# Head 0's operands built from the masks' own raw tile, mask rows turned straight into place, and a last stage with its middle tap on ScalarE, its low parts on VectorE and three gate buffers

## The reference

```python
# 1: attention within clusters, for each of 2 x 8 heads of 768 x 64
q_assign = argmax(q_n @ c_n.T); k_assign = argmax(k_n @ c_n.T)     # 16 centroids, rows normalised
mask = q_assign[:, None] == k_assign[None, :]
scores = where(mask, q @ k.T / 8, -1e9)
x = softmax(scores) @ v
# 2: Fourier mixing over tokens and channels, then a two-layer MLP on the normalised sum
u = x + real(fft(fft(x, axis=1), axis=2)); un = layernorm(u)
x = u + relu(un @ w_ch1) @ w_ch2
# 3: gated layer with a convolution of 3 taps along the tokens
h = relu(x @ w_in)                                                # 2 x 768 x 1024
conv_out = conv_w[0] * h_left + conv_w[1] * h + conv_w[2] * h_right
out = (h * sigmoid(conv_out)) @ w_out
```

## Time and profile before

| | us |
|---|---|
| runs | 730.78, 731.47, 728.44 (median 730.78) |
| profiled execution, its own time | 728.22 |
| its span, first to last instruction | 726.4 |
| TensorE busy | 704.0 (97% of the span) |
| VectorE, ScalarE, GpSimd busy | 378.1, 289.9, 286.4 |
| granted TensorE clock, mean | 0.991 of full speed |

### The profile page before, as it was taken

One profiled execution on the slowest core, in us unless ns is written; L12 is line 12 of the kernel. 1 busy time (PEld: TensorE's weight loads), 2 busy tenths in 40 slices (PEclk: granted clock), 3 DMA queues, 4 the chain that ended last, 5 costly groups with the idle time before them and its releaser, 6 DMA issues.

```text
span 726.4 us, 10339 instructions
## 1 busy us (share of the span) xinstructions
PE 704.0 (97%) x3927; PEld 631.5 (87%) x3927; DVE 378.1 (52%) x704; ACT 289.9 (40%) x602; POOL 286.4 (39%) x305
## 2 busy tenths in 40 slices
PE   8899999999999999999999999999999999799998
PEld 8799999999999999988888888888888899688886
DVE  3688778788888883973312311132111378874410
ACT  2567667676767773211002110021001264443320
POOL 3466697588548606067820000000041247531100
PEclk8899999999999999999999999999999999999999
DMA  5525445242435202133300000000040331000011
GB/s 164 142 79 131 127 102 144 62 104 62 128 121 153 63 1 66 30 76 103 112 30 1 0 1 1 0 29 30 0 162 12 110 95 30 0 30 16 28 49 54
DMA packets 26865, 48.09 MB, mean 66 GB/s; under 512 B 4032, under 2 KB 11456, under 8 KB 26560
## 3 DMA queue, kind: packets, MB, share of 16 engines
q1 hardware_dynamic: 24240, 39.44, 19.7%
q0 software_dynamic: 2448, 7.95, 3.4%
q10 hardware_dynamic: 128, 0.05, 0.0%
HBM read 36.41 MB, written 3.15 MB: 54 GB/s over the span
## 4 chain that ended last, share of the span: by engine, by line
PE 77%; DVE 10%; ACT 8%; issue 2%; POOL 1%; DMA 1%; SPq 0%; ACTq 0%; POOLq 0%
PE ps L1508 18%; PE ps L1474 18%; PE ps L1570 9%; PE ps L1273 8%; PE ps L1259 6%; PE ps L1556 5%; ACT prob L674 3%; PE ps L1247 3%; PE ps L1248 3%; PE ps L1214 3%; ACT pt_h L686 2%; DVE pt_l L870 2%; DVE gate L1165 2%; DVE row_min L863 2%; PE ps L1353 1%
## 5 line engine op out<-in xcount | busy, mean ns | idle before, releaser
L1103 DVE SCALAR_TENSOR_TENSOR hid_l<-ps,hid_h 128x512 fp32r<-128x512 f32 x48 | 33.2, 692 | 197.2 <-ACT hid_h L772 197.2
L870 DVE TENSOR_TENSOR pt_l<-ps,pt_h 128x384 fp32r<-128x384 f32 x192 | 101.0, 551 | 47.1 <-ACT pt_h L686 46.0
L772 ACT ACTIVATE hid_h<-ps 128x512 fp32r<-128x512 f32 x48 | 28.7, 598 | 223.7 <-PE ps L1474 223.7
L686 ACT ACTIVATE pt_h<-ps 128x384 fp32r<-128x384 f32 x192 | 84.0, 490 | 56.6 <-PE ps L1259 56.5
L863 DVE TENSOR_REDUCE row_min<-ps 128x1 f32<-128x768 f32 x96 | 90.3, 940 | 8.1 <-PE ps L1248 8.1
L1259 PE MATMUL ps<-cst,prob 128*128 128x128 f32 x576 | 82.3, 280 | 9.5 <-ACT prob L674 9.5
L674 ACT ACTIVATE prob<-ps,row_min 128x768 f32<-128x768 f32 x96 | 87.3, 909 | 5.3 <-DVE row_min L863 4.9
L1259 PEld LDWEIGHTS ps<-cst,prob 128*128 128x128 f32 x576 | 65.4, 144 | 18.7 <-ACT prob L674 14.7
L1508 PE MATMUL ps<-w_h,hid_h 128*128 128x512 f32 x192 | 76.2, 397 | 0.0
L1508 PE MATMUL ps<-w_h,hid_l 128*128 128x512 f32 x192 | 75.5, 393 | 0.0
L1508 PE MATMUL ps<-w_l,hid_h 128*128 128x512 f32 x192 | 74.7, 389 | 0.0
(11 more groups left out here) (166 smaller groups left out, 1570.3 us busy)
## 6 DMA issues: line engine op xcount, KB each, us to landing
w_raw<-in_moe_w_ch SPq DMA_DIRECT2D x24, 256.0 KB, 2.6
raw_d<-in_q SPq DMA_DIRECT2D x8, 384.0 KB, 3.9
raw_d<-in_k SPq DMA_DIRECT2D x8, 384.0 KB, 5.6
raw_qk<-in_q SPq DMA_DIRECT2D x16, 192.0 KB, 4.9
raw_qk<-in_k SPq DMA_DIRECT2D x16, 192.0 KB, 3.2
raw_v<-in_v SPq DMA_DIRECT2D x16, 192.0 KB, 2.5
q<-q SPq DMA_DIRECT2D x16, 192.0 KB, 4.4
k<-k SPq DMA_DIRECT2D x16, 192.0 KB, 4.1
```

Of the source, the lines that this page charges most:

```text
L686: nc.scalar.activation(pt_h[a][:, R * hf:R * hf + R, (t % R) * P:(t % R + 1) * P], ps[:, 4 + hf, 0:HALF].rearrange("p (j c) -> p j c", j=R ...
L870: nc.vector.tensor_tensor(pt_l[a][part], ps[:, 4 + hf, 0:HALF].rearrange("p (j c) -> p j c", j=R), as_f32(pt_h[a][part]), ALU.subtract).th ...
```

## The change

**Head 0.** No DMA copy and no mask DMA serves head 0 any more. q and k of head 0 are rows 0 to 63 of the masks' raw tiles, so they aren't loaded a second time: GpSimd scales `raw_d[0]` into `raw_qk`, ScalarE writes the high part twice (into `q1` and `q2`) and the same for k, GpSimd takes both low parts. The raw k tile is now issued at the start of ScalarE's queue. The mask rows of head 0 are turned by `turn_rows`, 6 transposes for q and 6 for k, straight to partitions 0 to 15 of PSUM; ScalarE copies q's rows and half of k's into place, VectorE the other half. `keep_busy(12)` and `keep_busy(8)` have become `keep_busy(2)` and `keep_busy(4)`. An exponential that nobody reads brings ScalarE's table load forward. The dots and the masks of unit 1 move one step later against the steps of head 0.

**Last stage.** The middle tap is an activation with a scale on ScalarE (`middle_tap`), all low parts are VectorE's, GpSimd only splits `w_out`, now right at the start, from four raw buffers loaded earlier and one DMA for the high part; `act_s` and `gate` have three buffers, sigmoid, gate and low part follow one and two rounds behind.

```diff
-                        if n or j == 0:
-                            sp.dma_start(as_f32(mask_place(t, tp)), as_f32(rows_of(n, j, tp))).then_inc(done, 16)
+                        sp.dma_start(as_f32(mask_place(t, tp)), as_f32(rows_of(n, j, tp))).then_inc(done, 16)
...
+            sp.dma_start(raw_d[0][:, :], pair_of(q_t, 0)).then_inc(raw_d_loaded[0], 16)
+            load_k(0, 1)
             load_v(0, 0)
             sp.dma_start(taps[:, :, :], conv_w).then_inc(taps_loaded, 16)
+            sp.wait_ge(q2_first, 1)
+            sp.wait_ge(q_split, 1)
+            load_q(0, 1)
+            sp.wait_ge(k_high, 1)
+            sp.wait_ge(k_split, 1)
+            load_dots(1)
...
+            serve(0, 1)
+            for i in range(1, PAIRS - 1):
...
-            scale_q(0)
-            split_qk(0, 0)
+            pool.wait_ge(raw_d_loaded[0], 16)
+            nc.gpsimd.tensor_scalar(raw_qk[0:D, :], raw_d[0][0:D, :], -SCALE, 1.0, ALU.mult,
+                                    ALU.mult).then_inc(q_scaled, 1)
+            pool.wait_ge(q_scaled, 1)
+            pool.wait_ge(q_high, 1)
+            low(q1[0][D:P, :], raw_qk[0:D, :], as_f32(q1[0][0:D, :])).then_inc(q_split, 1)
+            pool.wait_ge(q_split, 1)
+            pool.wait_ge(k2_first, 1)
+            low(k1[0][0:D, :], raw_d[1][0:D, :], as_f32(k2[0][0:D, :])).then_inc(k_split, 1)
...
+            nc.gpsimd.dma_start(out_h[:, :, :], w_out.rearrange("(f p) c -> p f c", p=P)).then_inc(outw_high, 16)
+            pool.wait_ge(mlp_ready, B * NT)
...
+            for t in range(3):
+                step(0, 0, t)
             store_mask(1)
-            for t in range(2, 4):
-                step(0, 0, t)
+            step(0, 0, 3)
...
+            def middle_tap(n):
+                act.wait_ge(relu_done, 2 * n + 2)
+                if n >= 3:
+                    act.wait_ge(g_low, n - 2)
+                nc.scalar.activation(gate[n % 3][:, :], act_s[n % 3][:, 1:S + 1], ACT.Copy,
+                                     scale=taps[:, 1, n % FT2:n % FT2 + 1]).then_inc(tap_done, 1)
...
             for n in range(B * FT2):
                 rectify(n)
+                middle_tap(n)
                 if n >= 1:
-                    gate_high(n - 1)
+                    squash(n - 1)
+                if n >= 2:
+                    gate_high(n - 2)
...
             for n in range(B * FT2):
+                convolve(n)
                 if n >= 1:
                     apply_gate(n - 1)
-                convolve(n)
-                if n >= 1 and not low_by_pool(n - 1):
-                    gated_low(n - 1)
-                if 1 <= n < FT2:
+                if n >= 2:
+                    gated_low(n - 2)
+                if n < FT2:
...
+            def turn_rows(j):
+
+                pe.wait_ge(mask_ready, j + 1)
+                for t in range(NT):
+                    last = nc.tensor.transpose(ps[0:C, 2 * j + t // R, t % R * P:(t % R + 1) * P],
+                                               mask_n[:, t // 2, t % 2, j, 0, :], ident)
+                last.then_inc(rows_turned, 1)
```

More of the change, by code:

```diff
@@ L50 @@
 ROW_LAG = 2
+RAW_OUT = 4
 def as_f32(ap):
@@ L167, in build @@
         out_h = sb(late, "out_h", [FT2, DM], F32R)
+        under = ExitStack()
+        out_raw = sb(under, "out_raw", [RAW_OUT, DM])
+        under.close()
+        g_l[1] = sb(late, "g_l1", [FT2, S], F32R)
         out_l = sb(late, "out_l", [FT2, DM], F32R)
-        g_h[0] = sb(late, "g_h0", [FT2, S], F32R)
         g_l[0] = sb(late, "g_l0", [FT2, S], F32R)
-        gate = [sb(late, f"gate{j}", [S]) for j in range(2)]
-        out_raw = sb(late, "out_raw", [2, DM])
+        gate = [sb(late, f"gate{j}", [S]) for j in range(3)]
+        act_s.append(sb(late, "act_s2", [S + 2]))
         out_s = sb(late, "out_s", [2, DM])
@@ L239, in build @@
         in_raw_loaded = [sem(f"in_raw_loaded{j}") for j in range(2)]
-        out_raw_loaded = [sem(f"out_raw_loaded{j}") for j in range(2)]
+        out_raw_loaded = [sem(f"out_raw_loaded{j}") for j in range(RAW_OUT)]
         xt_turned, xt_high, xt_low = sem("xt_turned"), sem("xt_high"), sem("xt_low")
@@ L635, in _ @@
-            for f in range(2):
-                split_out(f)
-            for n in range(B * FT2):
-                pool.wait_ge(relu_done, 2 * n + 2)
-                if n >= 2:
-                    pool.wait_ge(*low_done(n - 2))
-                nc.gpsimd.tensor_scalar(gate[n % 2][:, :], act_s[n % 2][:, 1:S + 1],
-                                        taps[:, 1, n % FT2:n % FT2 + 1], 1.0, ALU.mult,
-                                        ALU.mult).then_inc(tap_done, 1)
-                if n >= 1 and low_by_pool(n - 1):
-                    pool.wait_ge(g_high, n)
-                    low(g_l[0][:, n - 1, :], gate[(n - 1) % 2][:, :],
-                        as_f32(g_h[0][:, n - 1, :])).then_inc(g_low_pool, 1)
-                if n < FT2 - 2:
-                    split_out(n + 2)
+            nc.gpsimd.dma_start(out_h[:, :, :], w_out.rearrange("(f p) c -> p f c", p=P)).then_inc(outw_high, 16)
@@ L1028, in _ @@
             masks(1)
-            for t in range(1, 4):
+            for t in range(2, 4):
                 step(0, 0, t)
@@ L1164, in convolve @@
                         dve.wait_ge(conv_step, 2 * n + 1)
-                    nc.vector.scalar_tensor_tensor(gate[n % 2][:, :], act_s[n % 2][:, at:at + S],
-                                                   taps[:, tap, n % FT2:n % FT2 + 1], gate[n % 2][:, :],
+                    nc.vector.scalar_tensor_tensor(gate[n % 3][:, :], act_s[n % 3][:, at:at + S],
+                                                   taps[:, tap, n % FT2:n % FT2 + 1], gate[n % 3][:, :],
                                                    ALU.mult, ALU.add).then_inc(conv_step, 1)
@@ L1170, in apply_gate @@
                 dve.wait_ge(gate_done, n + 1)
[L1171 removed]
+                nc.vector.tensor_tensor(gate[n % 3][:, :], gate[n % 3][:, :], act_s[n % 3][:, 1:S + 1],
                                         ALU.mult).then_inc(gated, 1)
@@ L1333, in _ @@
                 dots(0, j)
-            keep_busy(12)
+            keep_busy(2)
+            turn_rows(0)
+            keep_busy(4)
+            turn_rows(1)
             turn_mask(0)
-            keep_busy(8)
-            dots(1, 0)
             scores(0, 0, 0)
             scores(0, 0, 1)
+            dots(1, 0)
+            step(0, 0, 0)
             dots(1, 1)
-            step(0, 0, 0)
             step(0, 0, 1)
+            step(0, 0, 2)
             turn_mask(1)
-            for t in range(2, 4):
-                step(0, 0, t)
+            step(0, 0, 3)
             for n in range(NH - 1):
```

144 lines of the change are left out of this document (76 added, 68 removed).

## The result

The changed kernel took 726.34 us (median of 20 runs, 721.54 to 728.74), the kernel before 729.38 us on the same chip (20 runs): a ratio of 0.9949, with a 95% interval of 0.9934 to 0.9963. Of the forecast 7.8 us, 3.0 came by the medians and 3.7 by the ratio. The profiled execution took 725.47 us, its span is 723.6 instead of 726.4.

The account below looks back on a forecast made before the run. TensorE, 97% busy, was taken to bound the kernel. Gains of 4.2 us from the start and 3.6 from the last stage, 7.8 in all, off the median 730.78 gave 723.0 us, range 719.5 to 728.0.

Parts of the forecast that it names:

- The likeliest case: Whole kernel: the forecast gains of start and last stage both come, 723.0 us, own range 720 to 725.5; chance 0.58.
- rival B: Head 1: TensorE's thin work lets the clock fall to half rate, costing 3.2 us, so 726.2 us; chance 0.17.
- First scores, 15.3: Start of head 0: first scores at 15.3 us instead of 20.02, 4.7 us earlier.
- price of 0.21 a record: Start of head 0: each filling matmul record or mask-row transpose was taken to last 0.21 us.
- From there to head 1, 16.1: First scores to head 1's: these come at 31.4 us, held by mask DMAs, instead of 35.63; gain 4.2 us.
- 27.5 for `mask_stored`: Head 0: masks of unit 1 stored at 27.5 us, head 1's scores following 3.9 us later.
- The last stage, 3.6: Last stage: 4.7 us of TensorE's waits vanish, less a new wait of 1.1; gain 3.6 us.
- the wait in narrow(0): Last stage, first `narrow`: TensorE waits 1.1 us for a late low part.
- the splits' delay: Last stage: GpSimd's splits of `w_out` hold VectorE up by 1.9 us, bounds 0 and 10.4.
- E: Last stage: VectorE's outer taps slow to 1.77 us each beside ScalarE, so the kernel gets slower, 736.7 us; chance 0.05.
- C: Last stage: `w_out` splits hold VectorE six times or more, 7.8 to 10.4 us; total 727.9 to 730.6; chance 0.12.
- D: Start: gives nothing, another transfer or low part replacing the mask DMA as head 1's limit; 727.2 us; chance 0.08.

Follow-up runs that it names:

- fill: Changed kernel plus matmuls nobody reads in head 0, four pairs ahead of `turn_mask(1)` and seven ahead of head 1's first scores: 725.27 us, ratio 0.9938.
- k_on_sp: Changed kernel with head 0's raw k tile issued behind raw q on SyncE instead of on ScalarE's queue: 725.55 us, ratio 0.9925.
- pool_masks: Changed kernel with head 1's two k mask DMAs issued from GpSimd's queue instead of SyncE's: 727.44 us, ratio 0.9952.
- start_only: Kernel before with only the head 0 half of the change: 727.36 us, ratio 0.9974.
- pieces: Changed kernel with the high part of `w_out` loaded in eight DMAs, each split waiting only for its piece: 726.14 us, ratio 0.9935.
- four_gates: Changed kernel with a fourth gate buffer: 722.86 us, ratio 0.9892.
- place_g: Changed kernel with only the SBUF places of `g_h[0]` and `g_l[0]` exchanged: 726.8 us, ratio 0.994.
- last_only: Kernel before with only the last stage's half of the change: 728.78 us, ratio 0.9982.
- swap_g: Kernel before with only the SBUF places of `g_h[0]` and `g_l[1]` exchanged: 729.95 us, ratio 1.0002.

## Why the prediction was right in kind and too large in size

Direction, both mechanisms and the places were right, and 726.34 lies in the range. "Faster by over 0.5%", which had a chance of 0.84, came by a hair: 0.9949, with the interval up to 0.9963. The likeliest case, 723.0, did not come. The result lies where rival B was put, 726.2, but that is luck: B's fall of the clock cost 1.6 us and not 3.2, and the larger part of the shortfall has other causes; besides, 726.2 was counted from a median of 730.78, and the kernel before now took 729.38. By the profiles the forecast gain of 7.8 has these parts (each from the table and the rows above):

- **First scores, 15.3.** 16.37, so 1.1 less. The filling behind the dots began at 10.00 and not at 9.61 (0.4), filling and mask rows took 5.26 to the start of `turn_mask` and not 5.05 (0.2), and from there to the first scores it took 1.11 and not 0.6 (0.5): k's rows take 0.55 on VectorE, and the first scores start only 0.36 us after them. What the prediction didn't see is that its price of 0.21 a record was itself read inside a stretch at 0.50, from 7.6 to 14.4 in the kernel before; at full clock a record takes 0.13 (fill, below). The changed kernel's profile had such a stretch of the same length in its start, so the price held; with a short one the same instructions bring the first scores at 15.04, near the forecast. The late centroids were not foreseen either; they are part of the first 0.4, with 0.25 us of idle, and k_on_sp, where they are early, starts its dots only 0.07 us sooner.
- **From there to head 1, 16.1.** Measured 16.10: the masks, not the steps, end last, and it is their DMAs, as pool_masks shows. The parts were off and cancel: 27.5 for `mask_stored`, set 1.07 late, would be 28.57 and was 28.13; the 3.9 from there to the scores were 4.34. The gain at head 1 is 3.16 instead of 4.2.
- **Rival B, 0.17.** It happened in six of the seven profiles that have the new start and no filling: the changed kernel, start_only, k_on_sp, pool_masks, pieces and four_gates. Its price of 3.2 was right for k_on_sp (3.0); in the others the stretch was half as long and cost 1.5 to 1.7. The argument against it ("from 32.60 to 34.99 it was no denser and nothing fell") was a fact about one execution: the seventh, place_g, shows the same instructions passing without a fall. The mean granted clocks of the changed kernel's 20 runs, 0.988 to 0.998, say that each had some lower clock, but not where. With the gap filled nothing fell there, in the one profile of each of three kernels.
- **The last stage, 3.6.** 1.18. Of the missing 2.4, the wait in narrow(0) is 0.9 (2.0, not 1.1), TensorE's other waits of the stage, of which none was forecast, are 0.5 (0.2 in `widen`, 0.3 for the transposes), and the place of `g_h[0]` is 0.8; 0.2 has no cause found. VectorE started where the forecast had it (585.74; 587.2 less the 1.6 won at the start is 585.6). Two terms behind that were too small: the splits' delay, taken as 1.9, was 1.25 + 1.94 + 1.09 = 4.3; and VectorE's idle for the tap, priced as the sigmoid's 0.84, is 1.07: the tap's 0.94 and two hand-overs. With that, and 0.87 from the gate's start to the low part's instead of 0.95, the round is 4.87, not 4.72. One was too large: this idle was counted from the first round on, but VectorE has none ahead of `convolve(1)`, `(2)` and `(3)`; the first two find their gates free, and low parts of the transposes fill the third. `convolve(9)` was due at 631.2 + 1.9 - 1.6 = 631.5 and came at 632.92. `narrow` at an unchanged 5.5 us was an assumption without a word: the diff moves its operand.
- **The other rivals.** E is dead: outer taps beside ScalarE take 1.03. C's mechanism is there at 4.3 us, not at 7.8. D is dead by head 1's first scores in start_only, 32.31 instead of 35.63.

Sum: 7.8 - 1.1 - 1.6 - 0.9 - 0.5 - 0.8 - 0.2 = 2.7, and the spans differ by 2.8. The medians differ by 3.0, and the ratio stands for 3.7.

## What to carry to other kernels

When a transfer moves to an idle queue, list what is in flight at that moment, here a small load that landed 1.3 us later; then look at what the chain behind it waits for, since TensorE had other work in all but 0.25 of the 1.3 us. Before a repair is credited with a gain, compare the stretches that it didn't touch: here they had moved by 1.5 us on their own, with the clock. When waits are cut out of a start that feeds TensorE thinly, price the clock with a chance, not with yes or no, and fill the gap with dead matmuls if a buffer is free. A rotation of n buffers whose refill waits for the last reader puts the refill in the reader's round; one more buffer was worth 2 us here, more than any other repair. And where a diff moves a tile in SBUF, its reader's pace is one of the terms.

## What the runs showed of the hardware

**The first matmuls are slow at a recorded clock of 1.00.** In fill, 20 records of the filling matmul took 4.61 us from 1.08 on, 0.23 each, and 8 of them 1.05 us at 24.54, 0.13 each; the granted clock reads 1.00 at both.

```profile
1.08 4.61 PE L1360 MATMUL ps<-cen_b 128*128 128x128 f32 x20 [1.08 <-POOL cen_b L483]
...
24.54 1.05 PE L1360 MATMUL ps<-cen_b 128*128 128x128 f32 x8
```

The Trainium skill, "TensorE: Matmul & The Clock Gate", section "What's actually happening", has half rate as the default state, which the paces agree with and the recorded column at the start does not. How long this lasts differs by execution. The 24 dots of the first unit took 2.86 us in k_on_sp and 5.30 to 5.33 in pool_masks, pieces, four_gates and last_only, where the record shows no fall before 20 us at all. In pieces the last six turns of mask rows still took 1.38 us, at 15.92 us and at a recorded 1.00, against 1.45 in the changed kernel at a recorded 0.50 and 0.82 in fill.

**The start of one profile can't be compared with that of another.** The changed kernel, fill, pool_masks, pieces, four_gates and place_g have the same instructions up to the first scores, and these come between 15.04 and 18.43 us: at 18.2 to 18.4 where the first matmuls are slow for long, at 16.37 where a stretch of 6.8 us at 0.50 is recorded, and at 15.04 where it is one of 3.4 us. The interval from one milestone to the next is the safer reading: from the first scores to head 1's the same six, pool_masks apart, differ by 0.05 us.

**The clock also falls in a stage that is otherwise full.** One wait of 2.0 us in narrow(0) was followed by a stretch near 0.50 in fill, pool_masks and place_g, which cost 1.3 to 1.6 us, and by none in the changed kernel. What decides stays open.

**The place of an operand in SBUF sets the pace of the matmuls.** 24 matmuls took 5.49 or 5.61 us by the place of `g_h[0]` (swap_g), and 5.56 where `g_h[0]` and `g_l[0]` had changed places (place_g). Which property of the address does it was not tried.
